# A fused linear attention, gated layer and expert layer: seven block products in place of eight in two thirds of the gate and value products

## What is computed

```python
n_tokens, d_model, d_ff = (1536, 512, 1536)

def _moe_ref(x, w_gate, w_val, w_out):
    g = x @ w_gate
    silu = g * (1.0 / (1.0 + np.exp(-g)))
    val = x @ w_val
    return (silu * val @ w_out).astype(np.float32)
```

## Time and profile before

| | us |
|---|---|
| median of 3 runs | 552.22 (551.95 to 552.44) |
| the profiled execution | 551.6 |
| its span, first to last instruction | 549.9 |
| PE busy in it | 541.5 |
| DVE, ACT, POOL busy in it | 316.7, 223.7, 74.7 |

### The profile page before, as it was taken

One profiled execution on the slowest core, in us unless ns is written; L12 is line 12 of the kernel. 1 busy time (PEld: TensorE's weight loads), 2 busy tenths in 40 slices (PEclk: granted clock), 3 DMA queues, 4 the chain that ended last, 5 costly groups with the idle time before them and its releaser, 6 DMA issues.

```text
span 549.9 us, 8573 instructions
## 1 busy us (share of the span) xinstructions
PE 541.5 (98%) x3255; PEld 459.3 (84%) x3255; DVE 316.7 (58%) x534; ACT 223.7 (41%) x359; POOL 74.7 (14%) x94
## 2 busy tenths in 40 slices
PE   8999999999999999999999999999999999999995
PEld 7888888888878888888788888778999999999994
DVE  7877455445455554453645667476676675766720
ACT  3115323323324343234233555266465554655511
POOL 5982000000000000000000020012220211202011
PEclk9999999999999999999999999999999999999999
DMA  8985531332213532323224554347764756655001
GB/s 299 320 280 204 186 114 62 112 116 66 108 60 113 149 105 111 114 63 108 89 102 140 172 201 149 163 157 273 267 225 165 272 186 247 214 169 203 1 27 35
DMA packets 18820, 84.49 MB, mean 154 GB/s; under 512 B 3421, under 2 KB 3421, under 8 KB 15201
## 3 DMA queue, kind: packets, MB, share of 16 engines
q1 hardware_dynamic: 13920, 71.35, 37.7%
q0 software_dynamic: 3712, 10.54, 5.5%
q10 hardware_dynamic: 1152, 2.13, 1.0%
HBM read 78.73 MB, written 7.39 MB: 157 GB/s over the span
## 4 chain that ended last, share of the span: by engine, by line
PE 96%; DMA 1%; issue 1%; SPq 0%; POOLq 0%; ACT 0%; POOL 0%; DVE 0%
PE bank L659 36%; PE bank L669 18%; PE bank L869 14%; PE bank L879 12%; PE bank L623 2%; PE bank L587 2%; PE bank L783 2%; PE bank L802 2%; PE bank L596 2%; PE bank L858 1%; PE bank L612 1%; DMA stage<-attn_in 1%; PE bank L695 1%; PE bank L912 1%; PE bank L680 1%
## 5 line engine op out<-in xcount | busy, mean ns | idle before, releaser
L1166 DVE TENSOR_TENSOR ewl<-stage,ewh 128x1024 fp32r<-128x1024 f32 x64 | 77.7, 1222 | 20.2 <-ACT ewh L956 20.1
L659 PE MATMUL bank<-xh,gvh 128*128 (+1 forms) x288 | 77.3, 390 | 0.0
L1287 DVE TENSOR_TENSOR sig<-bank,sig 128x512 f32<-128x512 f32 x36 | 24.8, 690 | 90.8 <-ACT sig L998 90.8
L659 PE MATMUL bank<-xh,gvl 128*128 (+1 forms) x288 | 77.0, 389 | 0.0
L659 PE MATMUL bank<-xl,gvh 128*128 (+1 forms) x288 | 77.0, 389 | 0.0
L956 ACT ACTIVATE ewh<-stage 128x1024 fp32r<-128x1024 f32 x64 | 66.9, 1054 | 1.1 <-DMA stage<-expert_w 1.0
L659 PEld LDWEIGHTS bank<-xh,gvl 128*128 128x128 f32 x288 | 54.1, 188 | 11.3
L659 PEld LDWEIGHTS bank<-xl,gvh 128*128 128x128 f32 x288 | 54.1, 188 | 11.3
L659 PEld LDWEIGHTS bank<-xh,gvh 128*128 128x128 f32 x288 | 53.8, 188 | 11.2 <-issue 0.2
L998 ACT ACTIVATE sig<-bank 128x512 f32<-128x512 f32 x36 | 21.5, 597 | 101.0 <-PE bank L659 101.0
L669 PE MATMUL bank<-hh,woh 128*128 128x512 f32 x144 | 57.3, 398 | 0.0
(11 more groups left out here) (184 smaller groups left out, 852.3 us busy)
## 6 DMA issues: line engine op xcount, KB each, us to landing
stage<-expert_w SPq DMA_DIRECT2D x28, 1024.0 KB, 4.9
stage<-mlp_w SPq DMA_DIRECT2D x36, 768.0 KB, 4.4
stage<-attn_in SPq DMA_DIRECT2D x24, 512.0 KB, 5.4
stage<-expert_w POOLq DMA_DIRECT2D x8, 512.0 KB, 5.8
x_rows<-x ACTq DMA_DIRECT2D x8, 260.0 KB, 5.0
x_rows<-x SPq DMA_DIRECT2D x4, 260.0 KB, 2.4
out<-ys,idx POOLq DMA_INDIRECT x16, 4.7
gx<-x_rows,idx POOLq DMA_INDIRECT x15
```

The source lines that it names most:

```text
L659: last = mm(bank[:, where, :], wt[:, k, :], (xh, xl)[x][:, k, bass.ds(g * GT, GT)], start=(at == 0), stop=(at == 3 * KD - 1))
L1166: V.tensor_tensor(dst, src, high.bitcast(F32), ALU.subtract).then_inc(inc, 1)
L1287: V.tensor_tensor(sig[:, :], bank[:, GATE_BANK, :], sig[:, :], ALU.mult).then_inc(sg_ready, 1)
```

## The change

In groups 0 and 1 the chunks are taken two at a time, as a pair `u` of 256 hidden features; pair 0 (chunks 0 and 1 of group 0) and the whole of group 2 stay as they were. For pairs 1 to 11, gate and value (`n` = 0, 1) are each a product of a 512x256 weight block and 512 tokens. It is cut in half three ways: model dimension, hidden features (the two chunks of the pair), tokens. Plainly that is eight block products; here it is Strassen's scheme in Winograd's form, with seven. Block products A11, A12 and A22 use weight blocks as they are; S1 to S4 use sums and differences of weight blocks, T1 to T4 of x blocks (`turnh`, `turnl`).

- POOL makes the four weight sums of a pair in float32 (`sum_weights`), the x combinations of a group once (`wholes`, `turns`: eight operations), and the low parts of the outward weights (`split_rows`).
- ACT and DVE split all seven weight operands of the next pair (`split_mix`), 128x512 each, and the four x operands of a group once (`split_turn`).
- PE runs `products(u)`: for each of the seven operands and each of n = 0, 1 six matmuls of 256 columns, into one half of a bank (4, 5 for the X sums, 6, 7 for the Y sums), accumulating on what stands there.
- In between ACT copies partial sums out (`keep`, three times two copies of 128x256), and DVE adds them back: `odd` (128x256, back into PSUM; A22 then accumulates on it) and `even` (128x512, to SBUF). The odd chunk of the pair is read from banks 4, 5, the even chunk from the `even` tiles.
- The outward products are as before, but come one pair later: PE's order is products(u), pair_out(u-1, 0), pair_out(u-1, 1).
- Loads of chunks come in pairs into four slots of 1536 columns. The loops over groups are written out. The end of group 0 is spread over pairs 7 to 10, its transposes between products and outward products. POOL's first loads of expert weights wait until pair 11's weights are read.

```diff
+            def whole(g, q):
+                kh, th = q // 2, q % 2
+                cols = slice(g * GT + th * HT, g * GT + (th + 1) * HT)
+                nc.gpsimd.tensor_tensor(xt[:, q, :, :], xh[:, kh * KH:(kh + 1) * KH, cols].bitcast(F32),
+                                        xl[:, kh * KH:(kh + 1) * KH, cols].bitcast(F32),
+                                        ALU.add).then_inc(whole_ready, 1)
...
+            def sum_weights(u):
+                def add(i, a, b, op):
+                    if u > 1:
+                        pool.wait_ge(mixl_ready, mixed(u - 1, i))
+                    nc.gpsimd.tensor_tensor(by_matrix(sums[i - S1][:, :]), a, b, op).then_inc(sums_ready, 1)
...
+                add(S1, quarter(u, 1, 0), quarter(u, 1, 1), ALU.add)
+                pool.wait_ge(sums_ready, (u - 1) * 4 + 1)
+                add(S2, mix_source(u, S1), quarter(u, 0, 0), ALU.subtract)
...
+            def products(u, free=None):
...
+                for i in range(MIXES):
+                    pe.wait_ge(mixl_ready, mixed(u, i))
+                    if i in turn:
+                        pe.wait_ge(turnl_ready, 4 * g + turn[i] + 1)
+                    for n in range(2):
...
+                        elif i in (S2, S4, S3):
+                            pe.wait_ge(kept_ready, held(u, i - S2, n))
+                        elif i == A22:
+                            pe.wait_ge(odd_ready, both(u, n))
...
+                        for w, x in split_terms:
+                            for k in range(KH):
+                                last = mm(where, mix(i, w)[:, n * KH * P + k * P:n * KH * P + (k + 1) * P],
+                                          moving[i][x][:, k, :], start=(first and at == 0), stop=True,
+                                          skip_group_check=True)
...
-            first_half(0)
+            gate_val(0, 1)
+            out_product(0, 0)
+            products(1)
+            out_product(0, 1)
...
+            for u in range(2, LAST_PAIR + 1):
+                products(u, banks_free(u))
...
+                pair_out(u - 1, 0)
+                if u == PAIRS + 1:
+                    turn_logits(0)
+                pair_out(u - 1, 1)
...
+            def keep(u, j, n):
+                act.wait_ge(prod_ready, product(u, (A11, S1, S2)[j], n))
...
+                    copy(kept[:, n, (0, 0, HT)[j]:(HT, 0, GT)[j]], bank[:, X_OF[n], 0:HT]).then_inc(kept_ready, 1)
...
+            unit(0, 0, None)
+            for t in range(4):
+                split_turn(0, t)
+            for i in range(2):
+                split_mix(1, i)
+            unit(0, 1, None)
+            for i in range(2, MIXES):
+                split_mix(1, i)
+            split_rows(1)
...
+            def pair(u):
+
+                more = u < LAST_PAIR
+                for i in range(4 if more else 0):
+                    split_mix(u + 1, i)
+                if u == PAIRS - 1:
+                    split_turn(1, T1)
+                    split_turn(1, T2)
...
+                for n in range(2):
+                    dve.wait_ge(prod_ready, product(u, S3, n))
+                    dve.wait_ge(kept_ready, held(u, 1, n))
+                    V.tensor_tensor(bank[:, X_OF[n], HT:], bank[:, X_OF[n], 0:HT], kept5[:, n, :],
+                                    ALU.add).then_inc(odd_ready, 1)
...
+                dve.wait_ge(pair_sig, both(u, 0))
+                V.tensor_tensor(even_sig[:, :], even[0][:, :], even_sig[:, :], ALU.mult).then_inc(pair_sg, 1)
```

More of the change, by code:

```diff
@@ L162, in bass_linear_attention_mlp_moe @@
         lt = sb("lt", [P, GT], F32, region2)
+        region3 = ExitStack()
+        sums += [sb(f"sums{i}", [P, GT], F32, region3) for i in range(2, 4)]
+        region3.close()
         exa = [sb(f"exa{i}", [P, KD, P], F32R, region2) for i in range(2)]
@@ L284, in bass_linear_attention_mlp_moe, with mix, by_matrix, quarter @@
         split_terms = ((0, 0), (0, 1), (1, 0))
+        woh += more_woh
+        wol += more_wol
+        hh += more_hh
+        hl += more_hl
+        Y_OF = (6, 7)
+        X_OF = (4, 5)
+        A11, S1, S2, S4, S3, A12, A22 = range(MIXES)
+        T1, T2, T3, T4 = range(4)
+        def mix(i, low):
+            if i < 4:
+                return (gvh, gvl)[low][i // 2][:, i % 2 * GT:(i % 2 + 1) * GT]
+            return (more_mixh, more_mixl)[low][:, i - 4, :]
+        def by_matrix(v):
+            return v.rearrange("p (n c) -> p n c", n=2)
+        def quarter(u, z, h):
+            return chunk_slot[u % 2 * 2 + z][:, 0:GV].rearrange("p (n h c) -> p h n c", n=2, h=2)[:, h, :, :]
+        def mix_source(u, i):
+            if i in (A11, A12, A22):
+                return quarter(u, int(i == A22), int(i != A11))
+            return by_matrix(sums[i - S1][:, :])
+        def out_rows(u, z):
+            return chunk_slot[u % 2 * 2 + z][:, GV:MW]
+        def pair_loads(u):
+            return (ATT_LOADS + u // 2 + 1) * 16
+        def mixed(u, i):
+            return (u - 1) * MIXES + i + 1
+        def product(u, i, n):
+            return (u - 1) * 2 * MIXES + 2 * i + n + 1
+        def both(u, n):
+            return (u - 1) * 2 + n + 1
+        def held(u, j, n):
+            return (u - 1) * 6 + 2 * j + n + 1
+        def mix_free(eng, u, i):
+            if u > 1:
+                eng.wait_ge(prod_ready, product(u - 1, i, 1))
+            elif i < 4:
+                eng.wait_ge(val_ready, i // 2 + 1)
         def flat(h):
@@ L422, in _, with wholes @@
                     fade(n)
+            def whole(g, q):
[4 more added lines that the diff above has]
+                                        ALU.add).then_inc(whole_ready, 1)
+            def wholes(g):
+                if g:
+                    pool.wait_ge(turnl_ready, 4 * g)
+                else:
+                    pool.wait_ge(xl_ready, 2 * GTT - 1)
+                for q in range(4):
+                    whole(g, q)
+                pool.wait_ge(whole_ready, 4 * g + 4)
@@ L424, in _, with split_rows @@
+            def split_rows(u):
+                for z in range(2):
+                    pool.wait_ge(pair_woh, both(u, z))
+                    at = (2 * u + z) % WO_BUFS
+                    nc.gpsimd.tensor_tensor(wol[at][:, :], out_rows(u, z), woh[at][:, :].bitcast(F32),
+                                            ALU.subtract).then_inc(pair_wol, 1)
+            wholes(0)
+            turns(0)
             pool.wait_ge(o_ready, NT)
@@ L442, in load_chunk @@
                 pool.dma_start(stage[2][:, half], expert_w[0, q][:, half]).then_inc(first_landed[j], 16)
+            for u in range(1, LAST_PAIR + 1):
+                sum_weights(u)
+                split_rows(u)
+                if u == 3:
+                    wholes(1)
+                if u == 4:
+                    turns(1)
+            pool.wait_ge(mixl_ready, mixed(LAST_PAIR, MIXES - 1))
+            pool.wait_ge(pair_wol, both(LAST_PAIR, 1))
             for j in range(2):
@@ L1410, in second_half @@
                          {HALF + 1: slots_a, NF1 - 2: rows_a}.get(f) if end else None)
-            first_half(0)
-            with dve.Fori(0, NG - 1) as g:
-                second_half(g)
-                first_half(g + 1, g)
+            unit(0, 0, None)
+            for t in range(4):
+                split_turn(0, t)
+            for i in range(2):
+                split_mix(1, i)
+            unit(0, 1, None)
+            for i in range(2, MIXES):
+                split_mix(1, i)
+            for u in range(1, LAST_PAIR + 1):
+                if u == PAIRS + 1:
+                    evacuate(0)
+                if u == PAIRS + 2:
+                    choose(0)
+                if u == PAIRS + 3:
+                    find_slots(0)
+                if u == PAIRS + 4:
+                    place_tokens(0)
+                    count_choices(0)
+                pair(u)
+            first_half(NG - 1, NG - 2)
             second_half(NG - 1, end=True)
```

321 lines of the change are left out of this document (276 added, 45 removed).

## The result

The changed kernel takes 566.05 us (median of 4 runs, 565.73 to 566.9), the kernel before in the same session 552.33 us. The ratio is 1.0252, with an interval of 1.0234 to 1.0270: 13.7 us slower, where 6.6 us faster was forecast (545.6, range 539.5 to 552.5). The profiled execution has a span of 563.9 us, 14.0 more than before.

What follows compares the result with a forecast made beforehand. PE was taken as the bound, busy 541.5 of 549.9 us. Saving 13.0 us on matmuls, less waits of 4.2 at pair 1 and 2.2 at pair 5, gave 6.6 us: median 545.6 us, range 539.5 to 552.5.

Steps and rivals of the forecast that it cites:

- 84 x 0.1155: PE's products of a pair: 84 short matmuls at the experts' price, 9.70 us instead of 10.88, saving 13.0 us over 11 pairs.
- bounds of 7 to 15: Range of PE's saving over 11 pairs: 7 us at 0.122 per short matmul, 15.0 us at 0.1133.
- that neither stretch shows: Closing caveat: prediction wrong altogether if something unseen in the pairs' old stretch or the experts sets matmul distance; no size.
- Rival (c): In the pairs' products, short matmuls with a wait for every six take 0.122 us each: 551.6 us; chance 0.06.
- 1.05 to 1.18 for 512: Duration in us of a POOL operation on 512 columns, giving 6.3 to 7.1 us of POOL work per pair.
- Ordinary pairs: 0: Pairs other than 1 and 5 make PE wait 0 us, even with DVE and POOL colliding.
- 0.6 us to the sigmoid's chain twice: At pair 1, DVE's six low parts meeting POOL's four sums add this, part of 2.9 us extra and 4.2 in all.
- its sums run while DVE has no deadline: POOL, working two pairs ahead, makes sums at 7.5 to 15 us in a pair, so ordinary pairs lose nothing.
- the sums in front of A22: At pair 5, six DVE low parts meet POOL's sums before A22: 1.6 us more, 2.2 in all.
- a fall of the granted clock: Clock dropping from 1.00 in PE's new waits, named as making the prediction wrong altogether; no size or chance given.
- (a): Rival: DVE and POOL don't disturb each other over long operations in the pairs, saving 11.1 us, 541.1 us; chance 0.32.
- (b): Rival: DVE and POOL exclude each other fully, about 1 us wait at A22 in ten pairs: 555.6 us; chance 0.11.

Runs made afterwards that it cites:

- rates2: Changed kernel with short matmuls varied in single pairs: one target bank (pair 3), cleared target per six (pair 6), no wait between sixes (pair 8); 565.52 us.
- the two fills: Changed kernel with each of POOL's sums, low parts and x combinations replaced by one fill (545.14 us) or three fills (550.25 us), which read no SBUF.
- the copy: Changed kernel with each of POOL's sums, low parts and x combinations replaced by a copy of one operand; 546.09 us.
- ungated: tuned2, but POOL makes the outward low parts without waiting for the pair's first odd addition; 556.85 us, 1.0076 to the kernel before.
- experiment 6: Four variants of the changed kernel with POOL's and DVE's work placed anew: tuned 550.27, tuned2 550.42, ungated 556.85, tuned3 549.33 us.
- tuned: Changed kernel: DVE makes weight sums, POOL's remaining work waits for the first odd addition, pair 1's operands reordered, `find_slots` split; 550.27 us, 0.9970 to the kernel before.
- rates3: Changed kernel with six or three long outward matmuls laid between the twelves of short ones in pairs 3, 10 and 11; 571.42 us.
- tuned2: tuned with DVE's queue shortened: outward low parts before sums, some pair 2 work behind pair 1's odd additions, `find_slots`' first step in pair 8; 550.42 us.
- rates: Changed kernel with term order, weight block or x block varied in pairs 10, 8, 11, and matmul marks in every second expert; 566.28 us.
- tuned3: tuned2 with pair 1 reordered on ACT, DVE's odd additions ahead of two low parts, and no POOL combination of x there; 549.33 us, 0.9952 to the kernel before.

## Why the prediction was wrong

**The matmul's price.** The step "84 x 0.1155" was mis-sized: 0.1199 measured, 10.07 us instead of 9.70, and with outward products of 5.47 instead of 5.44 a pair of 15.54 instead of 15.14. 8.6 us instead of 13.0, inside the bounds of 7 to 15. The row came from another stretch, and what sets the distance is something "that neither stretch shows", as the last sentence of the prediction feared. Rival (c)'s "products of 10.2 us" was nearly met, its reason (a wait for every six) was not: rates2 shows 0.120 without these waits.

**POOL's price.** The step "1.05 to 1.18 for 512" was too low; it was taken from multiplications by a decay table. Additions and subtractions of two full tensors take 1.29 alone and 1.62 to 1.75 beside DVE. The eight combinations of group 0's x were put at 8.4 us, ending at 52.3; they ended at 57.0, as POOL's timeline of the changed kernel shows, and so were still beside DVE's work on the first chunks:

```profile
49.11 7.90 POOL L557 TENSOR_TENSOR xt<-xt 128x512 f32<-128x512 f32 x4
```

**DVE beside POOL.** The mechanism was right, from one row of 0.69 beside 0.757, and it is shown by the two fills and the copy. The Trainium skill's rule (SBUF — State Buffer, "Who interferes with whom"), that a DVE instruction with two SBUF inputs contends with a GpSimd instruction that reads SBUF, and not with one that only writes it, agrees with all of them: 692 ns beside fills, 1.77 us beside sums, `even` with one input in PSUM at 685. Wrong was where it charged the meetings, and their size in pair 1. It took meetings at pairs 1 and 5 alone, "Ordinary pairs: 0", and PE waited for 17.0 us instead of 6.4.

Pair 1 cost 7.2 us instead of 4.2. The forecast added "0.6 us to the sigmoid's chain twice", and no wait in front of the first product. But the four turned low parts stand in DVE's queue ahead of chunk 1's sigmoid product, and beside POOL's sums they took 5.79 us, where four in a row take 2.5:

```profile
59.73 5.79 DVE L1535 TENSOR_TENSOR turnl<-xt,turnh 128x512 fp32r<-128x512 f32 x4
```

That gave the wait of 2.44 us at 67.46. Pairs 2 and 4, put at nothing, cost 2.7 and 3.6. The step that failed is "its sums run while DVE has no deadline": it places POOL's sums alone. POOL's two outward low parts are in its 6.3 us for a pair, but are placed nowhere, and the eight combinations of group 1's x are not counted at all. In pair 2 DVE was still late from pair 1, so that its last three low parts in front of A22 met the two outward low parts and took 4.06 us, where three in a row take 1.9 (DVE, then POOL):

```profile
93.38 4.06 DVE L1535 TENSOR_TENSOR gvl<-sums,gvh 128x512 fp32r<-128x512 f32 x3
```

```profile
93.81 3.07 POOL L587 TENSOR_TENSOR wol<-stages,woh 128x512 fp32r<-128x512 f32 x2 [1.51 <-ACT woh L1228]
```

In pair 4 it was the same with a sum in front. POOL had made four combinations of group 1's x from 97 to 103 us, and made the other four from 116 to 123. By the timeline they pushed its sums into DVE's way, DVE came late, and its three low parts took 5.13 us; no run moved these combinations alone:

```profile
116.14 6.86 POOL L557 TENSOR_TENSOR xt<-xt 128x512 f32<-128x512 f32 x4
```

```profile
128.59 5.13 DVE L1535 TENSOR_TENSOR gvl<-sums,gvh 128x512 fp32r<-128x512 f32 x3
```

```profile
129.79 3.39 POOL L587 TENSOR_TENSOR more_wol<-stages,more_woh 128x512 fp32r<-128x512 f32 x2
```

Pair 5 looks good (2.6 us, forecast 2.2), but in part by luck: the two turned low parts met the outward low parts at 148.39, not "the sums in front of A22", which came at 151.31. In pairs 3 and 6 to 10 the outward low parts began within 0.04 us of the first odd addition, so that DVE read PSUM beside them, and PE waited for no low part there, though some took up to 1.78 us. ungated in experiment 6 bears this out: letting these two operations alone run early raised the waits at A22 of pairs 2 and 5 from 0.71 and 0.23 us to 2.86 and 2.40.

**The clock.** The prediction named a fall of the granted clock as what would make it wrong altogether, and gave it neither a price nor a chance. It cost 4.7 us, a third of the loss. The kernel before has no matmul at the lower level, so its rows gave no price; the runs do: short matmuls 0.213 us apart instead of 0.120, long ones 0.427 instead of 0.227, 13 to 16 of them behind each of the three waits, 1.5 to 1.6 us each time.

**The small ones.** Pair 9's wait of 0.95 us behind `find_slots` was put at nothing. The end of group 0 costs 3.7 us more than plain pairs besides that wait, 3.84 forecast, and written-out loops cost nothing that a row shows: an undisturbed pair is exactly the sum of its matmuls.

**The rivals.** (a), no disturbance, is refuted. (b) had the mechanism, and with 555.6 the right side, at a chance of 0.11; but it spread about 1 us over ten pairs, and the waits at A22 came as 2.6 to 3.6 us in three pairs. The forecast and (b) differed only in where POOL's work falls, which was argued from the buffers of the sums alone. By the numbers that the runs gave, the sum is 8.6 - 17.0 - 0.5 - 4.7 = -13.6.

## What to carry to other kernels

Work given to an idle GpSimd is not free where VectorE reads two tensors from SBUF: cost each meeting with the whole operation of the other, list every operation of GpSimd's queue in order (also those that come once), and let those that read SBUF wait for a semaphore that VectorE raises when it turns to operands in PSUM; that one wait was worth 6.4 us here. Price a wait of TensorE of about 2 us and more with the matmuls that may follow at half the clock, here 1.3 to 2.8 us for each such wait. A matmul's distance is best taken from a stretch with the same operands and neighbours, or given a range of 5% that is carried into the result.

## What the runs showed of the hardware that was not expected

- A matmul of 256 columns with new weights goes at 0.120 us in the pairs, at 0.1155 in the experts, with the same shapes. Eight variations of operands, targets, waits and neighbours left it at 0.120, and a ninth in the experts left it at 0.1155.
- The length of a wait does not tell whether the clock falls. 3.43 us at 134.21 in the changed kernel and 1.91 at 77.40 in tuned had no sequel, 2.44, 2.51 and 2.41 in the changed kernel, 1.79 at 77.53 in rates3 and 1.88 in tuned2 had. Nor does the code in front of it: the same wait of 3.43 us in pair 4, by the same instructions in that pair, had a sequel in rates and in rates2 (granted clock 0.57 and 0.69 from 136 to 140 us), and there pair 5's 2.41 had none. So it can differ from one execution to the next, and a profile without a fall, as those of tuned and tuned3, need not stand for all runs. What decides it is open. The row in rates (columns as above):

```profile
136.00:140.00 4.00, 4.00 (x15) 3.27 (x14) 3.80 (x6) 2.62 (x6) 3.84 (x3) 0.57 0.00 0
```

- A GpSimd copy of one tensor holds VectorE's two-input operations as a sum of two does, for its shorter time.
- On GpSimd, a 128x512 sum of two tensors takes 1.29 us, a copy 0.62, a fill 0.53.
